# The experts' first weights in split form, moved over stationary token rows

## What is computed

```python
scores = where(block_i >= block_j, q @ k.T / sqrt(64), -1e9)     # attention, then rows of 512
# first mixture: N = 2304 rows, D = 512, E = 8 experts, F = 1024, capacity 576
e = argmax(x @ w_gate);  g = softmax(x @ w_gate)[e]
out = g * (relu(x @ w1[e]) @ w2[e])                # 0 for tokens beyond the capacity
# second mixture, for rows with x @ w_skip > 0, all others pass unchanged
out = x + g * (relu(x @ w1b[e]) @ w2b[e])
```

## Time and profile before

| | |
|---|---|
| median of three runs | 679.02 us |
| the profiled execution | 679.74 us, of which its span is 678.2 us |
| TensorE (PE) busy | 665.6 us, 98% of the span |
| VectorE (DVE), ScalarE (ACT), GpSimd (POOL) busy | 365.8, 266.2, 141.9 us |
| mean granted TensorE clock | 0.997 of full speed |
| share of the chain that ended last: `hidden` L1483, `values_of` L1491 | 34.0%, 25.6% |

### The profile page before, as it was taken

The page is one execution under the profiler, slowest core; times in us unless marked ns, Lnnn a source line. Parts: engine busy times, 40 slices in busy tenths (PEclk is TensorE's granted clock), DMA queues, the critical chain, the costliest instruction groups (busy, mean ns, idle before and its releaser), DMA issues.

```text
span 678.2 us, 16934 instructions
## 1 busy us (share of the span) xinstructions
PE 665.6 (98%) x5608; PEld 579.5 (85%) x5609; DVE 365.8 (54%) x1021; ACT 266.2 (39%) x657; POOL 141.9 (21%) x239
## 2 busy tenths in 40 slices
PE   7999999999999999999999999999999999999997
PEld 6888788887887889898899888888899899899996
DVE  2776877877787743367633367434711453411144
ACT  4556656656655122244422244123222352311233
POOL 5200012003003213322232112222122131112112
PEclk8999999999999999999999999999999999999999
DMA  9866559559515248210711148882364778701101
GB/s 185 198 172 194 142 165 260 155 129 274 131 27 182 71 115 304 69 33 24 263 56 31 47 167 313 307 318 78 128 236 163 277 278 311 266 31 48 45 18 34
DMA packets 95615, 105.90 MB, mean 156 GB/s; under 512 B 63757, under 2 KB 63757, under 8 KB 95568
## 3 DMA queue, kind: packets, MB, share of 16 engines
q1 hardware_dynamic: 84608, 81.03, 38.7%
q0 software_dynamic: 8912, 22.36, 10.2%
q10 hardware_dynamic: 2048, 1.87, 1.0%
HBM read 83.44 MB, written 28.63 MB: 165 GB/s over the span
## 4 chain that ended last, share of the span: by engine, by line
PE 95%; DVE 2%; issue 1%; DMA 1%; ACT 0%; DVEq 0%; POOL 0%; ACTq 0%; POOLq 0%
PE ps L1483 34%; PE ps L1491 26%; PE ps L1378 8%; PE ps L1329 7%; PE ps L1353 6%; PE ps L1385 4%; PE ps L1309 3%; PE ps L1321 2%; PE ps L1455 2%; PE ps L1461 1%; PE ps L1346 1%; PE ps L1469 1%; DMA kn<-in_k 1%; PE ps L1474 0%; PE ps L1334 0%
## 5 line engine op out<-in xcount | busy, mean ns | idle before, releaser
L1483 PE MATMUL ps<-xT,w 128*128 128x128 f32 x1344 | 159.4, 276 | 1.3 <-issue 1.0
L1483 PEld LDWEIGHTS ps<-xT,w 128*128 128x128 f32 x1344 | 155.1, 192 | 5.1 <-issue 3.0
L1491 PE MATMUL ps<-w_hi,hT_hi 128*128 128x512 f32 x256 | 104.6, 409 | 0.8 <-DVE hT_lo L1011 0.7
L1491 PE MATMUL ps<-w_lo,hT_hi 128*128 128x512 f32 x256 | 100.2, 392 | 0.0
L1491 PE MATMUL ps<-w_hi,hT_lo 128*128 128x512 f32 x256 | 99.7, 390 | 0.0
L1483 PE MATMUL ps<-xT,w_last 128*128 128x128 f32 x704 | 86.3, 277 | 0.3 <-issue 0.3
L1483 PEld LDWEIGHTS ps<-xT,w_last 128*128 128x128 f32 x704 | 82.3, 192 | 3.2 <-issue 2.5
L1214 ACT ACTIVATE hT_hi<-ps 128x512 fp32r<-128x512 f32 x64 | 38.0, 593 | 117.0 <-PE ps L1483 117.0
L1011 DVE SCALAR_TENSOR_TENSOR hT_lo<-ps,hT_hi 128x512 fp32r<-128x512 f32 x64 | 44.2, 690 | 63.9 <-ACT hT_hi L1214 60.4
L1152 ACT ACTIVATE probs<-ps,negmax 128x128 f32<-128x128 f32 (+3 forms) x128 | 65.9, 528 | 21.8 <-DVE negmax L762 21.8
L1209 ACT ACTIVATE w_hi<-w2all 128x1024 fp32r (+1 forms) x48 | 47.0, 1046 | 62.8 <-PE ps L1491 56.9
(11 more groups left out here) (182 smaller groups left out, 867.4 us busy)
## 6 DMA issues: line engine op xcount, KB each, us to landing
w2all<-in_moe_w SPq DMA_DIRECT2D x10, 2048.0 KB, 14.9
w<-in_moe_w SPq DMA_DIRECT2D x7, 2048.0 KB, 9.6
rows<-queue POOLq DMA_DIRECT2D x36, 257.0 KB, 3.1
w2all<-in_moe_w SPq DMA_DIRECT2D x16, 512.0 KB, 5.8
w<-in_moe_w SPq DMA_DIRECT2D x12, 512.0 KB, 4.1
w_last<-in_moe_w SPq DMA_DIRECT2D x3, 2048.0 KB, 10.0
qn<-in_q SPq DMA_DIRECT2D x32, 144.0 KB, 3.5
out<-pad SPq DMA_DIRECT2D x4, 1152.0 KB, 8.6
```

The source lines that it names most:

```text
L1483: last = mm(hTp[j // 4][:, j % 4, :], w1s[slot][:, c, j * P:(j + 1) * P], xT[:, c, :], start=(c == 0), stop=(c == DC - 1))
L1491: last = mm(yp, h_[:, j, :].bitcast(f32r), w_[:, j, :].bitcast(f32r), start=(j + n == 0), stop=(j == FC - 1 and n == 2))
```

## The change

- **The first product.** In all tiles but 0 and 1 of each phase, `hidden` gives way to `hidden_rows`: the transposed rows are split in two (`xT_hi` by ScalarE's `copy_x`, `xT_lo` by VectorE's new `split_x`) and are stationary; the first weights stand split as `w1_hi` (one buffer) and `w1_lo` (written over the loaded weights), and move with 512 columns, in fp32r, 4 chunks times 3 terms times 2 halves.
- **The turning.** The hidden values now come out as rows. ScalarE keeps them (`keep_h`, two pieces of 128x512), TensorE turns them with 8 transposes (`transpose_h`), ScalarE (`copy_h`) and VectorE (`split_later_h`) split them.
- **Order.** TensorE does a tile's second product one tile later: `tile(t)` is hidden rows of t, transpose of rows, transpose of finished rows, the values of tile t-1 with the logits between their quarters, the turning of t's hidden values, and the ranks. The last tile's values stand in the next phase's opening (behind four pieces of its `hidden`), or after the loop.
- **Splitting the first weights.** When the next tile is the first of its expert, ScalarE makes four chunks of `w1_hi` (128x1024) as `hidden_rows` releases them, VectorE subtracts chunk 0 and GpSimd chunks 1 to 3 (`split_w1`). For tile 2 of each phase VectorE does all four, after tile 1's `hidden`.
- **The table** gets one word for each tile with slots, expert numbers and flags (`finish_table`, made after tile 0's values are taken); the second weights have three slots and not four; each kind of weight has one semaphore for all loads; SyncE pads all eight regions of phase 0.

```diff
-                def tile(t, slot, late=False):
-                    pe.wait_ge(p.x_copied, t + 1)
-                    hidden(range(0, 4), slot)
...
+                def hidden_rows(t, slot):
+                    for c in range(DC):
+                        if c == 0:
+                            pe.wait_ge(p.w1_split, t + 1)
+                        else:
+                            pe.wait_ge(p.w1_rest_split, t * 3 + c)
+                        carry()
+                        for n, (x_, w_) in enumerate(((xT_hi, w1_hi[:, c, :]), (xT_hi, w1_lo[:, slot, c, :]), (xT_lo, w1_hi[:, c, :]))):
+                            for half in range(2):
+                                last = mm(hp[half], x_[:, c, :].bitcast(f32r), w_[:, half * (F // 2):(half + 1) * (F // 2)].bitcast(f32r),
+                                          start=(c + n == 0), stop=(c == DC - 1 and n == 2))
+                        last.then_inc(p.w1_used, 1)
+                def tile(t, slot):
+                    pe.wait_ge(p.x_split, t + 1)
+                    hidden_rows(t, slot)
+                    transpose_x(t + 2)
+                    if phase == 0:
+                        transpose_y(t)
+                    else:
+                        pe.wait_ge(p.y_copied, t)
...
+                    values_tile(t, logits_between if phase == 0 else None)
+                    transpose_h(t, 0)
+                    transpose_h(t, 1)
+                    if phase == 0:
+                        ranks_y(t)
```

VectorE's order in one tile:

```diff
+                def tile(t):
+                    with dve.If(word > NEW - 1):
+                        split_w1(slot1(word), t * 4 + 4, range(0, 1), p.w1_split)
+                    with dve.Else():
+                        dve.wait_ge(p.w1_hi_ready, t * 4 + 4 + DC)
+                        dve.sem_inc(p.w1_split, 1)
+                    split_x(t + 2)
+                    if phase == 0:
+                        route_begin(t)
+                    with dve.If((word & BOTH) > 0):
+                        split_w2(slot2(word), t * 4, range(4))
...
+                        find_begun(count2[:, 0:1])
+                        route_end(t)
+                    split_later_h(0, t * 2 + 1)
...
+                    finish_tile(t)
+                    split_later_h(1, t * 2 + 2)
```

ScalarE's order in one tile is `copy_next`, `split_w1`, `copy_x`, `copy_yT`, `keep_h` 0, `copy_lgT`, `keep_h` 1, `split_w2`, `router_exp`, `copy_h` 0 and 1. GpSimd's:

```diff
                         load_rows(row_of(t + RING), ds(t % RING, 1))
+                        split_w1(t + 1, pool.value_load(...))
                         if phase == 0:
                             scatter_values(t)
```

The opening of phase 1 on TensorE, and the opening of both phases on ScalarE:

```diff
+                    hidden(range(0, 4), 0)
+                    of_last["transpose"](total)
+                    of_last["values"](total, last_between)
+                    hidden(range(4, 6), 0)
+                    of_last["ranks"](total)
+                    of_last["transpose"](total + 1)
+                    hidden(range(6, 7), 0)
+                    of_last["chunks"](total + 1)
+                    hidden(range(7, FC), 0)
+                    of_last["logits"](total + 1)
...
+                relu(1, 0)
+                relu(1, 1)
+                act.wait_ge(p.table_ready, 1)
...
+                    split_w1(slot1(word))
...
                 copy_x(3)
```

More of the change, by code:

```diff
@@ L235, in attention_moe_moe_kernel @@
         pool_chain = sem("pool_chain")
[L237 removed]
+        dve_chains = [sem(f"dve_chain{i}") for i in range(5)]
         carried = sem("carried")
@@ L567, in scatter_values, with split_w1 @@
                     scatter(out, ys[:, 0:D], idxo[:, 0:1], N - 1, p.scattered)
+                def split_w1(t, word):
+                    with pool.If(word > NEW - 1):
+                        slot = ds(pool.snap((word >> 9) & 3), 1)
+                        if isinstance(t, int):
+                            pool.wait_ge(p.w1_used, 12)
+                        for c in range(1, DC):
+                            pool.wait_ge(p.w1_hi_ready, t * 4 + (4 + c + 1))
+                            g.tensor_tensor(w1_lo[:, slot, c, :].bitcast(f32r).unsqueeze(1), w1all[:, slot, c, :].unsqueeze(1),
+                                            w1_hi[:, c, :].unsqueeze(1), ALU.subtract).then_inc(p.w1_rest_split, 1)
+                    with pool.Else():
+                        pool.wait_ge(p.w1_hi_ready, t * 4 + 4 + DC)
+                        pool.sem_inc(p.w1_rest_split, DC - 1)
                 def scatter_out(t):
@@ L998, in _, with count_split, split_w2 @@
                                  lg2p[:, 0, E:E + 1])
-                def split_w2(slot, before, quarters=range(4), of=p):
+                def count_split(p):
+                    dve.sem_inc(p.h_split, 1)
+                    dve.sem_inc(p.w2_split, 4)
+                def split_w2(slot, before, quarters, of=p):
                     for n in quarters:
@@ L1006, in split_w2, with split_w1, split_x, split_later_h @@
                                           w2_hi[:, chunks, :].unsqueeze(1), ALU.subtract).then_inc(of.w2_split, 1)
-                def split_h(half, value):
+                def split_w1(slot, before, chunks, done, p=p):
+                    for c in chunks:
+                        dve.wait_ge(p.w1_hi_ready, before + (c + 1))
+                        vec.tensor_tensor(w1_lo[:, slot, c, :].bitcast(f32r).unsqueeze(1), w1all[:, slot, c, :].unsqueeze(1),
+                                          w1_hi[:, c, :].unsqueeze(1), ALU.subtract).then_inc(done, 1)
+                def split_x(value):
+                    dve.wait_ge(p.x_copied, value)
+                    vec.tensor_tensor(xT_lo[:, :, :].bitcast(f32r), xTp, xT_hi[:, :, :], ALU.subtract).then_inc(p.x_split, 1)
+                def split_later_h(half, value):
+                    dve.wait_ge(p.h_copied, value)
+                    hs = slice(4 * half, 4 * half + 4)
+                    vec.scalar_tensor_tensor(out=hT_lo[:, hs, :].bitcast(f32r), in0=later_hTp[half], scalar=0.0,
+                                             in1=hT_hi[:, hs, :], op0=ALU.max, op1=ALU.subtract).then_inc(p.h_split, 1)
+                def split_h(half, value, p=p):
                     dve.wait_ge(p.h_copied, value)
@@ L1210, in split_w2, with split_w1 @@
                                       ACT.Copy).then_inc(p.w2_hi_ready, 1)
-                def relu(t, half):
+                def split_w1(of, ahead=None, p=p):
+                    for c in range(DC):
+                        if ahead is not None:
+                            act.wait_ge(p.w1_used, ahead * 4 + (c + 1))
+                        sc.activation(w1_hi[:, c, :].bitcast(f32r).unsqueeze(1), w1all[:, of, c, :].unsqueeze(1),
+                                      ACT.Copy).then_inc(p.w1_hi_ready, 1)
```

535 lines of the change are left out of this document (321 added, 214 removed).

## The result

| | before | after |
|---|---|---|
| median | 679.03 us | 746.06 us (745.04 to 748.76, 4 runs) |
| ratio, 95% interval | | 1.0991 [1.0957, 1.1024] |
| profiled span | 678.2 us | 747.2 us |
| mean granted clock | 0.997 | 0.953 |

A forecast was written before the change was run, and what follows sets the result against it. TensorE, busy 98% of the span, was taken as the bound. Terms -21.3 + 12.6 + 3.2 + 9.8 + 1.0 + 3.0 - 1.5 + 5.2 = +12.0 us gave a 691.0 us median, range 673 to 704.

The forecast's parts named there:

- GpSimd's subtraction: First-weight split on GpSimd: 2.4 us each, hidden in phase 0, up to 1 us late in all in phase 1: +1.0 us.
- chunk 3 is read at 17.9: Phase 0 tile: GpSimd's three chunks end at 15.8 us, before chunk 3 is read at 17.9, so hidden.
- The rival at 721 us: GpSimd becomes the bound: at 4 us a chunk, 2.7 us late in each of 11 tiles, +30 us; chance 0.10.
- the clock's count: Clock falls after each of three waits of 5 to 6.6 us, 3.5 us at half speed each: +5.2 us.
- the opening of phase 1: Tile 1 to tile 2, phase 1: late table, tile 2 starts at Z + 42.0, stall 6.6 us.
- The tile gain: Later tiles, both phases: cheaper hidden_rows less added transposes, net -0.76 us a tile, -21.3 us over 28 tiles.
- a sign of being wrong: Later tiles: the prediction would be wrong if hidden_rows took more than 5.6 us.
- The waits for finished rows behind tiles that split second weights: Phase 0: VectorE finishes rows at 21.6 us, TensorE wants them at 19.6; 2.0 us waits, five tiles, +9.8 us.
- The seam: Between the phases: TensorE waits 0.9, 0.3 and 5.0 us, less 3.0 lost before: net +3.2 us.
- The end: After the loop: TensorE, ready at 12.3, waits for y_copied until VectorE finishes at 15.4: +3.0 us.
- `xT_lo` as the last thing before tile 2: Both openings: TensorE's gaps of about 6 us ahead of tile 2 are ended by VectorE's split_x, giving xT_lo.
- my other terms: All but GpSimd's: gain -21.3, openings +12.6, seam +3.2, splitting tiles +9.8, end +3.0, old stalls -1.5, clock +5.2 us.

The follow-up runs named there:

- VectorE doing all: The changed kernel with VectorE subtracting all four chunks of the first weights and GpSimd none: 1.0431 against the kernel before.
- the combination: The changed kernel with VectorE subtracting all first-weight chunks, ranks behind the next tile's first hidden-rows chunk, second weights' split behind finish_tile: 1.0436 against the kernel before.
- the early-chunks run: The changed kernel with ScalarE's four w1_hi chunks for tile 2 made ahead of tile 1's relus: 1.1002 against the kernel before.

## Why the prediction was wrong, and where it was right

**Failed: "GpSimd's subtraction", +1.0 us, and the reason given against its rival.** The length of one subtraction was right: 2.31 to 2.37 us alone, 2.4 forecast. GpSimd's own lateness was not: no wait in phase 0, as forecast, but 6.7 us in phase 1 where 1.0 stood. (The start that I took, 8.6 us, is more than its parts, 5.2 + 0.8 + 2.3; in tile 4 it was 9.75.) What failed above all is who pays. I priced only GpSimd's own lateness ("chunk 3 is read at 17.9"), and wrote against the rival that "nothing on VectorE that takes two inputs from SBUF runs for most of that stretch". Three operations of the routing do. They are 0.17 us each, and I had looked at their busy time, which is nothing, and not at what a wait of up to one GpSimd instruction does to a chain of 20 of them that TensorE awaits at the end of its tile. The earlier trace rows had the sign: a scatter beside VectorE's split took 1.90 us for 1.02. I used it to stretch GpSimd and not to stretch VectorE. The experiments show the size: 59 us for such instructions in the old kernel, where every later tile has them, and 38 us back when they leave the new one. The rival at 721 us named the right engine with the wrong mechanism: its price was for GpSimd at 4 us a chunk.

**Failed with it: the clock's count.** I counted three falls, after the three long gaps, and wrote that waits of 2 us should not do it. With waits in eight of the 15 tiles of phase 0's loop it falls six times more, the mean is 0.94, and that is 15 us of it. It fell behind the waits of 1.85 us in tiles 8 and 14 (0.50 granted from 370 to 373 and from 469 to 472), and not behind the waits of 1.82 and 1.80 us in tiles 6 and 13. The size of one fall was near: 1.4 to 2.8 us of work for 1.75.

**Missing: issue.** I had no term for TensorE's own restart. While matmuls are queued it runs ahead over the branches between experts. With the ranks as the last thing in a tile, and waiting, it can't: 1.6 us at each of three changes of expert, 0.8 at a fourth, 4.3 us at the jump, 10.0 us in all. It shrinks when the waits shrink (5.4 with VectorE doing all, 1.2 in the combination). The gaps are filled with the sequencer's reads of the table and branches, as shown above.

**Mis-sized: the opening of phase 1.** Forecast Z + 42.0, measured Z + 48.9. Of the 6.9 us, 2.0 lie ahead of the end of tile 1's `hidden` (541.3, that is Z + 36.9, for 34.95): the work at half the clock behind the seam's wait, which I had in another term. The rest has two causes that end within 0.2 us of each other, so neither can be charged alone: the load is issued 7.5 and not 3.4 us behind the last pad, and the table ends behind a scatter that takes until Z + 37.7 to land, where my whole count for it came to Z + 36.2 with 4 us of work behind the scatter. In phase 0 tile 2 started at 253.6 and not 251.5. ScalarE's chunks were done at 250.3 there and the rows came at 250.9, and the early-chunks run shows that without ScalarE's part the rows alone hold it as long.

**Right.** The tile gain: 13.76 and 12.36 us against 13.7 and 12.3, -19.4 us over 28 tiles where -21.3 stood; `hidden_rows` took 5.68 us at full clock, just over the 5.6 that I had named as a sign of being wrong. The waits for finished rows behind tiles that split second weights: 1.8 us in four of five, 2.0 forecast. The seam: 0.8 and 4.6 us for 0.9 and 5.0. The end: 3.9 for 3.0. `xT_lo` as the last thing before tile 2, 1.65 us behind the transposes. Without GpSimd's part and with these as they are, the forecast would have been right about the sign only: the kernel with VectorE doing all stands at 1.0431, some 30 us, where my other terms made 11. Of the 19 us between, 11 are in its loop of phase 0, which takes 229.8 us: 5.4 in issue, and TensorE busy for 216.2 us where 15 tiles need 206.4, at a mean clock of 0.96. The rest is spread over the two openings and phase 1.

Whether a GpSimd subtraction placed where VectorE has no two-input operation would be free was not tried.

## What to carry to other kernels

Before work goes to GpSimd, list VectorE's instructions with two SBUF inputs that can fall beside it, small ones above all, and price each at the length of the GpSimd instruction, not at its own; if one of them is in a chain that TensorE awaits, that is the price of the edit. A wait at the end of a tile can cost more than itself: TensorE's lead over its branches goes, and then the clock. When a product is moved away from an opening, ask what it covered there: here it was the landing of pads and rows.

## What was unexpected of the hardware

- A VectorE operation of 128x8 elements with two SBUF inputs takes until the running GpSimd instruction ends: 1.56 to 2.10 us in tile 4 (2.34 at most elsewhere) beside subtractions of 2.34 us, 0.17 alone. One with an operand in PSUM, or with one input, keeps its 0.17 us.
- A one-input GpSimd copy (1.10 us) does the same, for about its own length (1.26 us at most).
- Two large streams, VectorE's and GpSimd's, take about the sum of their times: 11.3 us for 4.63 and 7.01.
- TensorE restarted 1.6 us after a wait that stood ahead of a change of expert, and 4.3 us where two empty experts were passed over; 1.0 us for the same jump when it ran ahead. Each read of a table word by its sequencer takes 0.30 us.
- The granted clock fell to 0.50 behind two of four waits of 1.80 to 1.85 us.
